# First slices and units of a feed-forward pair moved into the last steps of a delta-rule scan

## What is computed

```python
state = zeros(B, H, D, D)                                  # B 4, H 8, D 48
for t in range(768):                                       # k_n: normalised keys
    y[t] = q[t] @ state
    state += beta[t] * outer(k_n[t], v[t] - k_n[t] @ state)
x = y as 3072 tokens of 384 features
h = x @ w_in                                               # 384 x 2048
P = a0 + a1*h + a2*h**2 + a3*h**3;  Q = 1 + |b0|*|h| + |b1|*h**2
x = (P / (Q + 1e-6)) @ w_out                               # 2048 x 384
x = (maximum(x @ w_in2, 0) ** 2) @ w_out2
```

## Time and profile before

| what | us |
|---|---|
| median of three runs | 1138.98 (1137.4 to 1139.11) |
| the profiled execution, its own time | 1141.11 |
| its span, first to last instruction | 1139.4 |
| mean granted TensorE clock | 0.987 |
| TensorE busy / weight loads busy | 1097.6 / 945.6 |
| VectorE / ScalarE / GpSimd busy | 681.8 / 654.3 / 507.5 |

### The profile page before, as it was taken

One profiled execution on the slowest core, in us unless ns is written; L12 is line 12 of the kernel. 1 busy time (PEld: TensorE's weight loads), 2 busy tenths in 40 slices (PEclk: granted clock), 3 DMA queues, 4 the chain that ended last, 5 costly groups with the idle time before them and its releaser, 6 DMA issues.

```text
span 1139.4 us, 18197 instructions
## 1 busy us (share of the span) xinstructions
PE 1097.6 (96%) x6352; PEld 945.6 (83%) x6352; DVE 681.8 (60%) x1120; ACT 654.3 (57%) x1307; POOL 507.5 (45%) x626
## 2 busy tenths in 40 slices
PE   8798999999978999999999999899999999999998
PEld 6598999999976788888888888788888888888886
DVE  6985566333349988888888888855343433334332
ACT  5664676654459877787777778654333433333332
POOL 5087887683009878777777777500000000000000
PEclk9898999999988999999999999999999999999999
DMA  8937887464533000010101003330100101010000
GB/s 190 204 75 159 163 164 165 94 123 84 128 96 104 15 24 33 1 56 1 56 1 56 1 0 112 96 113 14 48 8 1 56 1 56 1 56 1 1 28 28
DMA packets 173627, 74.42 MB, mean 65 GB/s; under 512 B 135968, under 2 KB 161696, under 8 KB 172576
## 3 DMA queue, kind: packets, MB, share of 16 engines
q1 hardware_dynamic: 163936, 68.54, 25.3%
q10 hardware_dynamic: 9600, 4.72, 1.6%
HBM read 52.27 MB, written 20.71 MB: 64 GB/s over the span
## 4 chain that ended last, share of the span: by engine, by line
PE 65%; DVE 4%; ACT 1%; issue 1%; ACTq 0%; DVEq 0%
PE ps_y L1108 11%; PE ps_y L1110 11%; PE ps_y L1109 11%; PE ps_h L1093 11%; PE ps_h L1095 11%; PE ps_h L1094 11%; DVE w_in_lo L1227 1%; DVE ps_h L1264 1%; DVE cubic L1242 1%; DVE ps_h L1248 0%; DVE w_out_lo L1230 0%; DVE g_hi L1257 0%; DVE g_lo L1272 0%; ACT w_in_hi L1131 0%; ACT coef L1151 0%
## 5 line engine op out<-in xcount | busy, mean ns | idle before, releaser
L1093 PE MATMUL ps_h<-x_hi,w_in_lo 128*128 128x512 f32 x576 | 227.3, 395 | 16.1 <-DVE g_lo L1272 7.4
L1094 PE MATMUL ps_h<-x_lo,w_in_hi 128*128 128x512 f32 x576 | 226.1, 392 | 0.0
L1095 PE MATMUL ps_h<-x_hi,w_in_hi 128*128 128x512 f32 x576 | 225.8, 392 | 0.0
L1108 PE MATMUL ps_y<-g_hi,w_out_lo 128*128 128x512 f32 x576 | 224.2, 389 | 0.1
L1109 PE MATMUL ps_y<-g_lo,w_out_hi 128*128 128x512 f32 x576 | 224.1, 389 | 0.0
L1110 PE MATMUL ps_y<-g_hi,w_out_hi 128*128 128x512 f32 x576 | 224.1, 389 | 0.0
L1283 DVE TENSOR_TENSOR q<-h_sq 128x512 f32<-128x512 f32 x96 | 66.3, 691 | 135.6 <-ACT h_sq L1172 134.0
L1093 PEld LDWEIGHTS ps_h<-x_hi,w_in_lo 128*128 128x128 f32 x576 | 109.4, 190 | 40.8 <-issue 9.3
L1179 ACT ACTIVATE g_hi<-q 128x512 fp32r<-128x512 f32 x96 | 60.7, 633 | 141.5 <-PE ps_y L1110 137.0
L1336 POOL TENSOR_SCALAR den_part<-h_sq,b_abs 128x512 f32<-128x512 f32 x96 | 73.8, 769 | 135.0 <-ACT h_sq L1145 134.7
L1352 POOL TENSOR_TENSOR head_times_q<-q,g_hi 128x512 f32<-128x512 f32 x96 | 124.6, 1298 | 10.9 <-DVE g_hi L1257 10.9
(11 more groups left out here) (101 smaller groups left out, 1926.0 us busy)
## 6 DMA issues: line engine op xcount, KB each, us to landing
kq<-kq_in SPq DMA_DIRECT2D x10, 768.0 KB, 5.4
shared<-w_in SPq DMA_DIRECT2D x32, 192.0 KB, 3.9
shared<-w_out SPq DMA_DIRECT2D x32, 192.0 KB, 4.4
vkp<-k_in SPq DMA_DIRECT2D x12, 384.0 KB, 4.7
vkp<-v_in SPq DMA_DIRECT2D x12, 384.0 KB, 5.9
iq<-kq_in SPq DMA_DIRECT2D x12, 384.0 KB, 4.5
x_first<-y_t ACTq DMA_DIRECT2D x24, 192.0 KB, 2.9
shared<-x_first SPq DMA_DIRECT2D x6, 768.0 KB, 5.9
```

The costliest lines, as they stand in the source:

```text
L1093: pe.matmul(bank(n), lo, x_hi[:, slot, k, :], start=(k == 0), stop=False)
L1094: pe.matmul(bank(n), hi, x_lo[:, slot, k, :], start=False, stop=False)
L1095: mm = pe.matmul(bank(n), hi, x_hi[:, slot, k, :], start=False, stop=(k == KT - 1))
L1108: pe.matmul(ps_y[m][:, :], lo, g_hi[:, d, :], start=(f == 0), stop=False)
```

## The change

Scan and layers become one block; the layers' functions are called from within the scan's loops.

- SyncE: the cross loads of quad h stand first in step 4h-3 (before: later in the step, for h = 2 at step 6). `load_blocks(r)` moves to one step later and behind `store_inverse`. The feed-forward loads start at step 36 instead of 42 and still wait for the last stored inverse; in steps 38 to 47 one more slice is loaded each, after the slice four before it is split.
- ScalarE and VectorE split slices 0 to 9 in steps 37 to 46, and the three parts of the first x tile in steps 39, 41 and 43. A slice is one copy and one subtraction of 768 columns instead of two of 384.
- TensorE: up(0) after step 46, up(1) and up(2) within step 48; ScalarE takes h of units 0 and 1 in steps 47 and 48, and makes the reciprocal of unit 0. After the scan TensorE waits for the copy of the last y and goes on at unit 3. VectorE does head(0) right behind polynomial(0) and rest(0) and g_lo(0) one unit later, instead of two and three; GpSimd does its product of unit 0 right behind its denominator.
- Slices 10 to 15 of layer 1 are split beside units 7 to 12, as before. Slices 0 to 2 of layer 2 are split at units 89, 91 and 93.
- The last tile's output is stored with three DMAs, one behind each copy.
- Buffers: the scan's tiles and the layers' share memory; the layers use the scan's PSUM banks, up banks 7, 0, 1, 2, 5 and down banks 3, 4, 6.

```diff
+    FF_LOADS, FF_SPLIT, FF_X = GROUPS - 12, GROUPS - 11, (39, 41, 43)
@@ SyncE
             for n in range(LAST_MM):
+                for h in range(2, QUADS):
+                    if n == 4 * h - 3:
+                        load_cross(h)
...
-                for r in range(2, ROUNDS):
-                    if n == step_of_quad(2 * r + 1):
-                        load_blocks(r)
-                for h in range(2, QUADS):
-                    if n == max(4 * h - 3, INV_OUT[h // 2]):
-                        load_cross(h)
                 for r in range(1, ROUNDS):
                     if n == INV_OUT[r]:
                         store_inverse(r)
+                for r in range(2, ROUNDS):
+                    if n == step_of_quad(2 * r + 1) + 1:
+                        load_blocks(r)
...
-                if n == GROUPS - 6:
+                if n == FF_LOADS:
                     sp.wait_ge(inv_stored, 16 * (ROUNDS - 1))
-                    moe_inputs.load_first(sp, x_out)
+                    ff.load_ab(sp)
+                    ff.load_weights(sp, 0)
+                    ff.load_x(sp, 0)
+                    for i in range(1, ff.W_SLOTS):
+                        ff.load_weights(sp, i)
+                if 0 <= n - FF_LOADS - 2 < ff.PRE:
+                    ff.load_weights(sp, n - FF_LOADS - 2 + ff.W_SLOTS)
+            ff.sync(sp)
@@ GpSimd
             for r in range(1, ROUNDS):
                 invert(r)
+            ff.gpsimd(pool)
@@ TensorE
                 if n >= 2:
                     y_and_state(n - 2)
+                if n == GROUPS:
+                    ff.up(pe, 1)
...
+                if n == GROUPS - 2:
+                    pe.wait_ge(n_ready, len(ACT_N))
+                    pe.wait_ge(p_ready, GROUPS - UPFRONT)
+                    ff.up(pe, 0)
+                if n == GROUPS:
+                    ff.up(pe, 2)
+            pe.wait_ge(y_ready, GROUPS)
+            ff.tensor(pe)
@@ ScalarE
                     take_z_first(n)
+                if n in FF_X:
+                    ff.split_x_hi(act, FF_X.index(n), 0)
...
+                if 0 <= n - FF_SPLIT < ff.PRE:
+                    ff.split_weights_hi(act, n - FF_SPLIT)
+                if n == GROUPS - 1:
+                    ff.take_h(act, 0)
+                if n == GROUPS:
+                    ff.guess_recip(act, 0)
+                    ff.take_h(act, 1)
+            ff.scalar(act)
@@ VectorE
+                if n == FF_SPLIT:
+                    ff.coef_bounds(dve)
+                if 0 <= n - FF_SPLIT < ff.PRE:
+                    ff.split_weights_lo(dve, n - FF_SPLIT)
+                if n in FF_X:
+                    ff.split_x_lo(dve, FF_X.index(n), 0)
+            ff.vector(dve, ys_done, GROUPS)
@@ the layers
+    W_SLOTS, W_AHEAD, PRE = 4, 3, 10
+    EARLY = {UNITS - 7: 0, UNITS - 5: 1, UNITS - 3: 2}
...
+    def scalar(act):
+        for n in range(2, ALL + LAG_RECIP):
+            f, tile = n % FT, n // FT
+            if n in EARLY:
+                split_weights_hi(act, FT + EARLY[n])
+            if n < ALL and n % UNITS < FT and f + W_AHEAD < FT and (n >= UNITS or f + W_AHEAD >= PRE):
+                split_weights_hi(act, n // UNITS * FT + f + W_AHEAD)
...
+    def vector(dve, ys_done, groups):
+        for n in range(ALL + LAG_LOW):
+            if 1 <= n - LAG_HEAD < UNITS:
+                head(dve, n - LAG_HEAD)
...
+            if n == 0:
+                head(dve, 0)
+            if n == 1:
+                rest(dve, 0)
+                dve.wait_ge(ys_done, groups)
+                low_of_ratio(dve, 0)
...
+        last = 2 * TILES - 1
+        for k in range(KT):
+            sp.wait_ge(out_read, KT * last + k + 1)
+            sp.dma_start(y_dram[1][:, k, bass.ds((TILES - 1) * TN, TN)], y_tile[:, k, :]).then_inc(out_stored, 16)
```

More of the change, by code:

```diff
@@ L1 @@
+from collections import namedtuple
 from contextlib import ExitStack
@@ L110, in build_attention @@
[L110 to L117, removed]
+        quads = [room.take(QUAD).rearrange("r (g p d) -> r g p d", g=4, p=PAIRS)
+                 for room in (first_x, common, common, second_x, late, late, late, late)]
@@ new lines, in build_attention @@
+        kq = late.take(4 * QP * C, D2).rearrange("r (s a q c) -> r s a q c", s=2, a=2, q=QP)
+        k_diag = late.take(16 * PAIRS * BL, D2).rearrange("r (s g f h t) -> r s g f h t", s=2, g=2, h=2, t=BL)
+        prod = [first_x.take(BL * BL // 4) for _ in range(2)]
+        upper = common.take(BL * BL).rearrange("p (j i) -> p j i", j=BL)
+        before = common.take(C)
+        beta, sq_sum, root, norm, key_beta = (common.take(GP) for _ in range(5))
+        cross = late.take(8 * PAIRS * WIDE).rearrange("p (g q i) -> p g q i", g=8, q=PAIRS)
@@ L949, in build_moe_pair, with build_feed_forward @@
[L949 to L954 removed]
+                if n == FF_SPLIT:
[5 more added lines that the diff above has]
+            ff.vector(dve, ys_done, GROUPS)
+def build_feed_forward(nc, ctx, rows, moe_in, moe_out, coef_dram, memory, banks, x_first, x_second, out):
+    KT, FT, TN, TILES = rows["KT"], rows["FT"], rows["TN"], rows["TILES"]
@@ new lines, in build_feed_forward, with deep @@
+    x_hi, x_lo = x_split[:, :, 0], x_split[:, :, 1]
+    ab, b_abs = memory["ab"], memory["b_abs"]
+    room = Room(memory["common"])
+    def deep(count):
+        return room.take(count * TN).rearrange("p (s n) -> p s n", s=count)
+    h_sq, b0_h, coef, den_part, cubic = (deep(SHORT) for _ in range(5))
+    q = deep(DEEP)
+    log_q = room.take(TN)
+    guess = deep(TRIPLE)
+    prod = deep(SHORT)
+    g_hi = memory["g_hi"].rearrange("p (s n) -> p s n", s=DEEP)
+    g_lo = memory["g_lo"].rearrange("p (s n) -> p s n", s=TRIPLE)
@@ new lines, in sync, with up @@
+        sp.wait_ge(out_stored, 16 * (last + KT))
+    def up(pe, n):
+        f, tile = n % FT, n // FT
+        slot, layer = tile % 2, n // UNITS
+        former = n - H_BANKS
+        if former >= UNITS:
+            pe.wait_ge(h_taken, former + 1)
+        elif former >= 0:
+            pe.wait_ge(g_lo_ready, former + 1)
+        if n % UNITS < FT:
+            pe.wait_ge(w_lo_ready, layer * FT + f + 1)
+        for k in range(KT):
+            if f == 0:
+                pe.wait_ge(x_lo_ready, KT * tile + k + 1)
+            hi = weights[:, f, k * P:(k + 1) * P]
+            lo = weights[:, f, 2 * D_MODEL + k * P:2 * D_MODEL + (k + 1) * P]
+            pe.matmul(bank(n), lo, x_hi[:, slot, k, :], start=(k == 0), stop=False)
+            pe.matmul(bank(n), hi, x_lo[:, slot, k, :], start=False, stop=False)
+            mm = pe.matmul(bank(n), hi, x_hi[:, slot, k, :], start=False, stop=(k == KT - 1))
+        mm.then_inc(h_ready, 1)
@@ new lines, in down @@
+    def down(pe, n):
+        f, tile = n % FT, n // FT
+        d, s = n % DEEP, n % TRIPLE
+        pe.wait_ge(g_lo_ready, n + 1)
+        for m in range(KT):
+            if f == 0 and tile > 0:
+                pe.wait_ge(out_read, KT * (tile - 1) + m + 1)
+            hi = weights[:, f, D_MODEL + m * P:D_MODEL + (m + 1) * P]
+            lo = weights[:, f, 3 * D_MODEL + m * P:3 * D_MODEL + (m + 1) * P]
+            pe.matmul(ps_y[m], lo, g_hi[:, d, :], start=(f == 0), stop=False)
+            pe.matmul(ps_y[m], hi, g_lo[:, s, :], start=False, stop=False)
+            mm = pe.matmul(ps_y[m], hi, g_hi[:, d, :], start=False, stop=(f == FT - 1))
+            if f == FT - 1 and m < KT - 1:
+                mm.then_inc(out_ready, 1)
+        mm.then_inc(down_done, 1)
```

760 lines of the change are left out of this document (333 added, 427 removed).

## The result

| | before | after |
|---|---|---|
| median of four runs | 1138.19 (1136.38 to 1139.11) | 1122.69 (1118.42 to 1124.61) |
| the profiled execution, own time / span | 1141.11 / 1139.4 | 1118.42 / 1116.7 |
| mean granted clock | 0.987 | 0.992 |

The ratio is 0.985, with a 95% interval of 0.9835 to 0.9865 (the two medians alone give 0.986): faster, by 15.5 us in medians. The forecast was 22 less. The profiled execution of the changed kernel was the fastest of its four, so profile against profile shows 22.7, which flatters the change. Both facts matter: the profiled execution agrees with the forecast's sum, and the median does not.

What follows compares the result with a forecast made beforehand. TensorE bounds the kernel, busy 1097.6 of 1139.4 us. Transition -8.3, first g_lo -6.5, first tile -1.1, between layers -4.9, end -0.8, scan shift -0.5 sum to -22.1: 1117 us, forecast band 1114 to 1120, range 1109 to 1125.

Steps and rivals of the forecast that it cites:

- rival 2: Steps 37 to 40: feed-forward loads go first, TensorE waits over 4 us, its clock falls; 1121 to 1125; chance 0.18.
- s: Shift of the scan against the kernel before: taken as -0.5 us, bounds -5 and +4.
- the wait for the last y's copy: After the scan, before up(3): TensorE waits 0.7 us, bounds 0.2 and 2.5.
- The term for the splits in the scan: Late scan steps: splits fit ScalarE's and VectorE's free time and cost nothing, as long as their data is there.
- The boundary between the layers: Before up(96): with slices split early nothing holds it; -4.9 us, bounds -4.9 and -3.
- the first tile: Units 7 to 12: the remaining 2.3 us become about 1.2; -1.1 us, bounds -2.3 and 0.
- the reserve for slow subtractions: First tile: if all six wide splits were slow beside GpSimd, none of the 1.1 us would be gained.
- the end: Last store: carries 256 KB instead of 768; -0.8 us, bounds -1.2 and +0.5.
- the scan up to step 38: Step 7: 4.3 of 4.8 us of kq wait go; step 8 starts at 105 to 107 instead of 111.1.
- E: End of GpSimd's round 5, its last: 262.3 instead of 266.75, bounds 260.5 and 267.5.
- slice 0: Step 37: in at E + 9.5, ScalarE wants it at E + 6.4; TensorE stands about 2.4 us.
- step (c): From E to step 40: quad 10's loads land by E + 19.5 to E + 21; TensorE waits 1 to 2.7 us.

Runs made afterwards that it cites:

- experiment 5: Against the changed kernel: layer 2's slices 0 to 2 split at unit 96, not at units 89, 91 and 93; 1125.26 us, ratio 0.9869.
- experiment 10: Against the kernel of experiment 2: the last tile's output stored by one DMA instead of three; 1116.04 us, ratio 0.9797.
- experiment 1: The changed kernel run again with no edit; 1121.46 us, ratio 0.9834.
- experiment 2: Against the changed kernel: quad 10's loads go ahead of slices 2 and 3 and the first x tile, x split later; 1112.98 us, ratio 0.9769.

## Why the prediction was right or wrong

*Right: the time.* 1122.69 lies in the range (1109 to 1125) and the sign is right, but it is 5.7 above the number. It is in the band of rival 2 (1121 to 1125) and not in that of the forecast (1114 to 1120). Two of the bands don't follow from their own terms: 1112.5 less 0.8, 1.2 and 0.4 is 1110.1 and not 1109, and s = +3 to +6 gives 1120.5 to 1123.5 and not up to 1125. The measured time lies inside either way.

*Right: every term behind the scan.* Up(3) was put at 333.7 for s = 0 and came at 333.71; the wait for the last y's copy was 0.47 (taken 0.7). g_lo(0) started at 335.31 and made no wait; g_lo(1) left 0.97 (0.8). The term for the splits in the scan, nothing by itself, held as far as their data was there. From up(3) to the last matmul there are 3428 pitches; 779.43 - 3428 x 0.227 = 1.3 is left of what was 14.3. The boundary between the layers shows no wait at all and full pitch; this is up(96) and the down behind it:

```profile
711.15 0.39 PE L1109 MATMUL ps<-x_split,weights 128*128 128x512 f32 x1
...
713.19 0.39 PE L1123 MATMUL ps<-g_hi,weights 128*128 128x512 f32 x1
```

Undoing that one part cost 3.2 in the profile and 3.8 between medians (experiment 5), against 4.9 taken. Of the profile pair's 13.0, 6.3 and 2.1 are waits for g_lo with the clock behind them, which leaves 4.6 for the boundary; some 1.6 of it was clock, which did not fall behind the wait of experiment 5.

*Too small: the first tile.* g_lo waits there fell by 2.1, not 1.1; the reserve for slow subtractions was not needed. Of the six wide subtractions beside GpSimd one took 1.58 and the median is 0.945, as in the scan. It is GpSimd that is slower beside them: its first denominator operation (L1327) has a median of 0.70 and took 1.41 to 2.11 in the six units with a split (VectorE by line, then GpSimd by line and one row of its timeline):

```profile
L1233 DVE TENSOR_TENSOR weights<-shared,weights x6: 943/945/1579, 350.2 to 372.8; 128x768 fp32r<-128x768 f32 x6
```

```profile
L1327 POOL TENSOR_SCALAR common<-common,b_abs x96: 687/697/2112, 325.2 to 710.0; 128x512 f32<-128x512 f32 x96
```

```profile
363.56 2.11 POOL L1327 TENSOR_SCALAR common<-common,b_abs 128x512 f32<-128x512 f32 x1
```

The section of the Trainium skill that the prediction quotes ("GPSIMD Engine Reference", section 1 Specifications) speaks of contention with such an instruction, and the trace agrees; it does not say that VectorE is the one that pays, and that step of the prediction was wrong. The price fell mostly on GpSimd, up to 1.4 us an operation; TensorE waited for a g_lo once in these units, for 0.23. *Too small: the end*, by 0.6: 1.4 instead of 0.8, beyond the bound of 1.2; experiment 10 confirms the cause.

*Right, in the first profile: the scan up to step 38.* `kq` was issued at 92.11 (91.7), step 8 started at 105.2 (105 to 107), GpSimd's round 2 at 100.92 (101) and its last at 222.56 (223.5); E was 261.24 (262.3). Timeline of ScalarE and GpSimd, for the earlier trace rows:

```profile
97.56 0.72 ACT L629 ACTIVATE scan_late<-scan_late,scan_common 96x512 f32<-96x512 f32 x1 [1.19 <-DMA scan_late<-kq_in]
```

```profile
100.92 2.37 POOL L394 TENSOR_TENSOR shared<-shared,scan_common 128x1024 f32<-128x1024 f32 x1 [7.13 <-DMA shared<-blocks]
```

*Half right: slice 0.* ScalarE's wait for it was put at such a length that TensorE would stand 2.4. The slice was there at E + 6.8, not E + 9.5: its halves landed in some 2.5 us, where the 4.4 of the earlier trace rows had been taken, a median over all 32 loads of this kind. TensorE stood hardly at all, ScalarE 1.0 (in the profile of experiment 1 it was 1.4 and 2.5):

```profile
268.00 0.84 ACT L1146 ACTIVATE weights<-shared 128x768 fp32r<-128x768 f32 x1 [1.03 <-DMA shared<-w_out]
```

But as step 40 hangs on E and the queue, that gain too ran into the same wait.

*Wrong: step (c), the shift s.* The place and the mechanism were right: step 40 starts when quad 10's loads are in, at E + 20.3 to 22.3 in four profiles (19.5 to 21 was given), at the late end of the band or past it, as the ring order of the Trainium skill has it ("DMA: Bandwidth & Descriptors", section "Queues, rings and completion order"). That these loads stand behind 2.3 MB of others is the cause, as experiment 2 shows; how the queue works through them inside is not taken apart here. Since slice 0 held little, TensorE was there 16.5 behind E, not 18.3, and since the queue held more, its wait was 3.8 to 5.2, not 1 to 2.7. And what the forecast left to a rival was in every one of these executions: behind the wait the clock fell, for another 1.7 to 3.2 us. s was 0 in the fastest execution and 6 in one of the slowest, against -0.5. That 0 is luck in part: step 40 came 1.1 earlier than forecast (281.55 against 282.7), and the clock took 1.7 that the sum had at nothing. In the median execution s was about 4, if it differs from the fastest one only there, as the two profiles do: that is the term of the sum that was mis-sized. One of the forecast's own marks against it, a step 40 after 286, was met in the slow execution (286.25), and not in the fast one.

*A choice of measure.* The sum was made against one execution, 2.1 above the median of its kernel, and met with one that lies 4.3 below the median of its own. Profile against profile it was 22.1 forecast and 22.7 measured, and that hid the error of s; only the repeat of experiment 1 showed it. These are the 5.7 by which the number was missed: 4.3 and 2.1, less 0.6, but for rounding. No run takes apart what made the profiled execution of the kernel before 2.1 slow.

What stays open: why the store of GpSimd's last round goes out between 261.2 and 264.7 in three profiles of the changed kernel's scan order and queue (the first, the one of experiment 1 and the one of experiment 5). The start of the scan differs already (step 2 at 63.8 in the first profile, 65.5 in the repeat), but no run here takes that apart. Open too is how much of a gain at step 7 is lost at step 40.

## What to carry to other kernels

When loads of the next stage go on the queue of the running one, issue what the running stage still needs first: three loads moved were worth 8.5 us here, as much as the early units (7) or more. A wait that another chain sets (a slower engine's end plus a queue) ends when that chain ends, 20.3 to 22.3 behind its store in four profiles here, so look for the last such point before summing gains that lie ahead of it. Judge by the median of several executions, and find out where in the range the profiled one lies. Where an engine changes stage, give the longest dependent chain a start of a few units, and price a wait of the matmul engine with its clock behind it, not only by its length.

## What the runs showed of the hardware

Behind waits of TensorE of 3.37, 3.78, 3.81, 3.93, 4.92 and 5.21 us the granted clock was 0.50 to 0.69 in windows of the next 2 to 5 us, and the work there took 1.5 to 3.2 us more than at full clock; behind waits of 2.77, 2.86 and 2.91 it stayed full. But between the layers it had fallen once after 3.13, and in the second profile of the kernel of experiment 2 behind a wait of 2.73, at the very place of the 2.77 (timeline of TensorE in step 9, then a window):

```profile
116.93 0.53 PE L566 MATMUL ps<-scan_common 96*96 96x96 f32 x4 [2.73 <-ACT scan_common L675]
```

```profile
118.00:120.00 2.00, 2.00 (x12) 2.00 (x11) 1.26 (x2) 0.61 (x3) 1.76 (x4) 0.50 1.02 149
```

So the same kernel at the same wait kept its clock once and lost it once: these rows make no rule of length, and a wait of nearly 3 us can cost more than itself. Issues alone slow down when the queue is full: the four inverse loads of quad 10, 64 KB each, took 3.03 to issue in the kernel before, 4.67 to 6.19 behind 2.3 MB (four profiles), and 3.65 to 5.03 behind the first two slices (eight profiles).
